# The next head's first scores stand between the third and the fourth turning group of an attention slot

## The reference

```
# q, k, v: 4 batches, 8 heads, 576 positions, 64 wide;  s: 4 x 8 x 576
cum    = cumsum(max(s, 0))
scores = q k^T / 8 + min(-(cum_i - cum_j), 0), causal
attn   = softmax(scores);  o = attn v                  # per head
x = o, heads side by side                              # 2304 tokens x 512
h = x w_in;  solu = h * softmax(h)                     # 2304 x 1024
y = layernorm(solu) * g_ln @ w_out                     # 2304 x 512
out = max(y w1, y w2, y w3) @ w_out2                   # 768 hidden units
```

## Time and profile before

| | |
|---|---|
| median of 3 runs | 727.67 us (727.65 to 728.1) |
| the profiled execution | 727.19 us, span 725.4 us |
| TensorE busy | 705.0 us, 97% of the span |
| VectorE, ScalarE, GpSimd busy | 382.7, 318.4, 258.3 us (53%, 44%, 36%) |
| granted TensorE clock | 0.999 of full speed |
| attention stage | from the start to about 212 us |

### The profile page before, as it was taken

One profiled execution on the slowest core, in us unless ns is written; L12 is line 12 of the kernel. 1 busy time (PEld: TensorE's weight loads), 2 busy tenths in 40 slices (PEclk: granted clock), 3 DMA queues, 4 the chain that ended last, 5 costly groups with the idle time before them and its releaser, 6 DMA issues.

```text
span 725.4 us, 12009 instructions
## 1 busy us (share of the span) xinstructions
PE 705.0 (97%) x4032; PEld 622.3 (86%) x4032; DVE 382.7 (53%) x681; ACT 318.4 (44%) x754; POOL 258.3 (36%) x298
## 2 busy tenths in 40 slices
PE   4899999999999999999999999999999999999998
PEld 3789899888888898989899998888888888888897
DVE  7999999999958656363635545410320132032121
ACT  4889999998964434141414414311211121111121
POOL 8767799999889554342202000000000000000000
PEclk9999999999999999999999999999999999999999
DMA  6577777778575142800000031001000000100000
GB/s 186 159 217 213 205 197 197 196 195 229 144 176 124 43 88 48 215 1 1 1 1 1 3 113 59 0 1 59 0 1 30 29 1 1 58 1 0 30 30 30
DMA packets 57721, 59.52 MB, mean 82 GB/s; under 512 B 23060, under 2 KB 44692, under 8 KB 57652
## 3 DMA queue, kind: packets, MB, share of 16 engines
q1 hardware_dynamic: 57684, 59.02, 30.4%
HBM read 44.15 MB, written 10.10 MB: 75 GB/s over the span
## 4 chain that ended last, share of the span: by engine, by line
PE 84%; DVE 6%; ACT 3%; POOL 3%; issue 3%; DMA 0%; DVEq 0%; POOLq 0%; ACTq 0%; SPq 0%
PE ps L687 10%; PE ps L689 10%; PE ps L688 10%; PE ps L492 6%; PE ps L603 5%; PE ps L605 5%; PE ps L604 5%; PE ps L528 4%; PE ps L530 4%; PE ps L529 4%; PE ps L705 3%; PE ps L707 3%; PE ps L706 3%; PE ps L474 3%; PE ps L500 2%
## 5 line engine op out<-in xcount | busy, mean ns | idle before, releaser
L689 PE MATMUL ps<-x_lo,w_hi 128*128 128x512 f32 (+1 forms) x360 | 132.4, 368 | 0.0
L688 PE MATMUL ps<-x_hi,w_lo 128*128 128x512 f32 (+1 forms) x360 | 132.4, 368 | 0.0
L687 PE MATMUL ps<-x_hi,w_hi 128*128 128x512 f32 (+1 forms) x360 | 132.4, 368 | 0.0
L888 ACT ACTIVATE probs<-ps,nmax 128x576 f32<-128x576 f32 (+4 forms) x160 | 82.8, 537 | 4.5 <-DVE nmax L1090 4.4
L492 PE MATMUL ps<-ident,probs 128*128 128x128 f32 x480 | 75.9, 283 | 5.9 <-DVE pt_lo L1097 2.7
L1097 DVE TENSOR_TENSOR pt_lo<-ps,pt_hi 128x512 fp32r<-128x512 f32 (+2 forms) x128 | 76.2, 636 | 7.9 <-ACT pt_hi L898 5.0
L689 PEld LDWEIGHTS ps<-x_lo,w_hi 128*128 128x128 f32 x360 | 67.9, 189 | 11.3
L688 PEld LDWEIGHTS ps<-x_hi,w_lo 128*128 128x128 f32 x360 | 67.9, 189 | 11.3
L687 PEld LDWEIGHTS ps<-x_hi,w_hi 128*128 128x128 f32 x360 | 67.9, 189 | 11.2
L898 ACT ACTIVATE pt_hi<-ps 128x512 fp32r<-128x512 f32 (+2 forms) x128 | 68.0, 560 | 12.6 <-PE ps L492 9.9
L474 PE MATMUL ps<-k_a,q_a 128*128 128x288 f32 (+2 forms) x192 | 63.4, 338 | 10.4 <-DMA qk_b<-setup 9.8
(11 more groups left out here) (103 smaller groups left out, 1420.6 us busy)
## 6 DMA issues: line engine op xcount, KB each, us to landing
qk_raw<-in_qk_dram SPq DMA_DIRECT2D x32, 576.0 KB, 4.1
xT<-halves SPq DMA_DIRECT2D x32, 144.0 KB, 2.4
xb_dram<-halves SPq DMA_DIRECT2D x32, 144.0 KB, 2.4
xb<-xb_dram SPq DMA_DIRECT2D x24, 192.0 KB, 3.7
rinvB<-rsum_dram SPq DMA_DIRECT2D x24, 192.0 KB, 4.5
stage<-in_moe_w_dram SPq DMA_DIRECT2D x18, 256.0 KB, 4.6
out_dram<-stage SPq DMA_DIRECT2D x18, 256.0 KB, 2.0
v_raw<-in_v_dram SPq DMA_DIRECT2D x32, 128.0 KB, 3.4
```

The lines of the kernel that those rows point to most:

```text
L687: pe.matmul(dst, w_hi[f][:, i, c, :], x2_hi[par][:, c, 0:w], start=(c == 0), stop=False)
L688: pe.matmul(dst, w_lo[f][:, i, c, :], x2_hi[par][:, c, 0:w], start=False, stop=False)
L689: mm = pe.matmul(dst, w_hi[f][:, i, c, :], x2_lo[:, c, CT * g:CT * g + w], start=False, stop=(c == KC - 1))
L888: act.activation(dst, SCORES[c], ACT.Exp, bias=nmax[par][:, c:c + 1], accum_out=sums_all[:, c, bass.ds(t, 1)]).then_inc(exp_done, 1)
```

## The change

S4 now stands between T2 and T3. Its waits for q's high part, k's high part, q's low part, the bias rows and the exp are gone from its head, which keeps only the wait for k's low part (slot 0's own first call and the call for head 1 keep more). Two of those left out, for q's and k's high parts, are implied by the low parts; the other three now stand inside T2, one ahead of each of its second, third and fourth blocks.

```
@@ turn
                 for n, (j, c) in enumerate(blocks):
                     o = chunk_offset(c) + P * j
+                    if g == 2 and n == 1 and live(known, -1):
+                        pe.wait_ge(exp_done, NCH * t + 1)
+                    if g == 2 and n == 2 and live(known, -1):
+                        pe.wait_ge(aux_loaded[1 - par], (t + par) * 8 + 16)
+                    if g == 2 and n == 3 and live(known, -1):
+                        pe.wait_ge(q_lo_ready, t + 2)
                     mm = pe.transpose(ps[:, GBANK[g], P * n:P * (n + 1)], probs[1 - par][:, o:o + P], ident[:, :])
@@ scores_4
-                pe.wait_ge(q_hi_ready, t + 1)
-                pe.wait_ge(k_hi_ready, t + 1)
-                pe.wait_ge(q_lo_ready, t + 1)
                 pe.wait_ge(k_lo_ready, t + 1)
-                pe.wait_ge(aux_loaded[par], (t - par) * 8 + 16)
+                if known is not None and known <= 1:
+                    pe.wait_ge(q_lo_ready, t + 1)
+                    pe.wait_ge(aux_loaded[par], (t - par) * 8 + 16)
                 if known == 0:
                     pe.wait_ge(q_b0_ready, 1)
-                else:
+                elif known == 1:
                     pe.wait_ge(exp_done, NCH * (t - 1) + 1)
@@ slot
                 if live(known, 1):
                     turn(2, t, par, known)
+                if live(known, -1):
+                    scores_4(t + 1, 1 - par, known and known + 1 if known != 0 else 1)
+                if live(known, 1):
                     turn(3, t, par, known)
-                if live(known, -1):
-                    scores_4(t + 1, 1 - par, None)
                 if live(known, 2):
                     values(t, par, 7, PV_B)
```

## The result

The changed kernel takes 740.6 us (740.23 to 740.89), the kernel before 727.66: a ratio of 1.0176, interval 1.0164 to 1.0188, 1.8% slower. The profiled execution has a span of 738.4 us against 725.4, 13.0 more. All of it arises in the attention stage: T0 of slot 3 moves from 29.12 to 29.50, T0 of slot 31 from 199.47 to 212.49. That is 182.99 us for 28 slots, where 170.35 stood.

A forecast was written before the change was run, and what follows sets the result against it. It took T0 to be held by ScalarE's exps, so a later T3 lengthens the slot to 6.35 us: 25 ordinary slots + 8.5, long ones - 0.5, sum + 8.0, giving 735.7 us, range 730.5 to 741.8.

The forecast's parts named there:

- What sets a slot: Attention stage: T0, the next slot's first turning, is held by ScalarE's exps, by 0.09 us; ScalarE has nothing to give.
- The loop, term by term: ScalarE loop from T0 to next T0: 2.84 + 1.08 + 0.54 + 1.86 = 6.32 us, 6.35 with the three waits.
- T0 to T2: TensorE from the first turning's start to the third's: 2.84 us, all of it matmuls back to back.
- T3 to its copy: From the start of turning T3 on TensorE to the start of its pt_hi copy on ScalarE: 0.54 us.
- Copy to T0: From the start of T3's copy on ScalarE, through three exps, to the next slot's T0: 1.86 us.
- the prediction's own sign of being wrong in size: The size would be wrong if T2 with its waits takes more than 0.5 us (among other signs).
- Three waits inside T2: Waits moved between T2's blocks: all for things long done, costing only issue time, 0.03 us for the three.
- waits dear: Rival: the three waits inside T2 cost the full 0.22 us, slot 6.54, total 741.0 us; chance 0.10.
- The six waits at S4's head: The gap ahead of S4's first load: six waits cost 0.22 us together, some 0.04 each.
- Ordinary and long slots: 25 ordinary slots become 6.35 us each, + 8.5; three long ones, 20.10 together, give - 0.5; sum + 8.0.
- GpSimd: It paced the slots in which it also splits w_in, at 6.12 us; these take the new 6.35 too.
- VectorE's longer loop: Rival: from T2 through T3's copy, pt_lo and q_low, 6.15 us, deciding if q_low exceeds 1.4; 741.2; chance 0.07.

The follow-up runs named there:

- e4: The changed kernel with ScalarE doing the three exps ahead of the copy of T3; 740.5 us, ratio 1.0177 against the kernel before.
- e1: The changed kernel with the wait for exp of chunk 4 back at S4's head, not inside T2; 735.37 us, ratio 1.0108 against the kernel before.
- e9: The changed kernel with two waits inside T2 swapped: q_a's low part ahead of the second block, exp of chunk 4 ahead of the fourth; 736.62 us.
- e2: The kernel before with S4 moved ahead of T3 and nothing else, all six waits at S4's head; 737.23 us, ratio 1.0131.
- e6: The kernel before, S4 behind T3, with ScalarE doing the three exps ahead of the copy of T3; 743.27 us, ratio 1.0213.
- e8: The kernel before with ScalarE's exps ahead of the copy of T3 and VectorE's q_low one head further ahead; 729.07 us, ratio 1.0018.
- e7: The changed kernel with exp wait at S4's head, ScalarE's exps ahead of T3's copy, VectorE's q_low one head further ahead; 726.11 us, ratio 0.9988.

## Why the prediction came out as it did

The direction and the loop that sets the slot were right: 735.7 was forecast, in 730.5 to 741.8, with 0.87 on slower; 740.6 came.

- **What sets a slot.** Right for the changed kernel: in its loop slots T0 comes 0.13 to 0.15 behind the last accumulator read and 0.92 to 0.96 behind VB's last matmul. For the kernel before it was read from one slot, and holds in ten of the 24 loop slots. In the other fourteen, all of slots 18 to 27 among them, T0 comes 0.11 or 0.12 behind VB's last matmul, which is TensorE's own pace; in slots 18 to 27 the last read ends 0.16 to 0.22 earlier. ScalarE had some 0.1 us to give there at most, too little to change the sum. e4 shows the hold of the exps as a cause: with the exps freed from the copy of T3, T0 follows VB by 0.11.
- **The loop, term by term.** T0 to T2: forecast 2.84, measured 2.83. S4: 0.66, measured 0.68. T3 to its copy: 0.54, measured 105.79 - 105.26 = 0.53. Copy to T0: 1.86, measured 107.62 - 105.79 = 1.83. T2: forecast 0.42 + 0.03 for the waits, measured 0.62. The sum is 6.49, and only one term was mis-sized. That is the prediction's own sign of being wrong in size, T2 with its waits above 0.5.
- **The term that failed** is "Three waits inside T2. All three are for things long done", and "They cost only issue time", with 0.03. One of them is not for a thing long done. I took from the order on ScalarE that exp of chunk 4 precedes the others and did not set its end beside the new place of the wait. It ends about 3.1 us after T0 (104.22 - 101.13); S4 needs it 3.2 after T0 (e1), but the second block of T2 asks for it at 2.9 already. The gap of 0.19 made the slot 6.50 instead of 6.29, 5.2 us in all (e1). That e1's 735.37 is so near the 735.7 that was forecast is in part luck: without the gap the ordinary slots are 6.29 where 6.35 was forecast, and the long ones and the start make up for it. The time of *waits dear*, 741.0, was nearly hit, but not for its reason: e9 has as many waits and no gap.
- **The six waits at S4's head.** Their 0.22 was read as a price of 0.04 each. e9 shows that a satisfied wait has no fixed price, and the same six cost 0.07 to 0.10 behind T2 (e2), but 0.17 to 0.23 behind T3 in nearly every loop slot of the kernel before, e6 and e8. That T3 had itself just been released from a wait would be a reason, but in three slots of e8 its loads follow T2's without a gap (seven in 0.76 and 0.80), and the gap ahead of S4 is still 0.17 or 0.18. In the one at 56.58 pt_lo of T1 ended at 56.98, only just ahead of T3's first load, so this doesn't settle it; the cause stays open.
- **Ordinary and long slots.** 25 x 6.35 was forecast; they came at (182.99 - 6.52 - 13.97) / 25 = 6.50, + 12.2 instead of + 8.5. The three intervals that were long sum to 6.52 + 13.97 = 20.49 instead of 20.10: one fell to the ordinary length, the two near the end grew. I had - 0.5. Another 0.4 came ahead of slot 3. So of the miss, 3.75 lie in the ordinary slots, 0.9 in the long ones and 0.4 ahead of them.
- **GpSimd** lost its role, as foretold: the slots that were its own are 6.50 like the others.
- **VectorE's longer loop** did not close in the changed kernel: q_low's median fell from 1.21 to 0.76. In e4 and e6 a loop through VectorE closes at 6.42, but another one than was priced: the copy of T3 hangs there on the exps and not on T3. Which loop is next behind ScalarE's in the changed kernel, no run shows.

## What to carry to other kernels

Filling a gap on the busiest engine gains nothing when the work pushed back feeds another engine that has no slack: follow the pushed instruction through the in-order queue of the engine that consumes it, back to where the first engine waits next, and add up that loop. A wait that is moved forward must be held against the time at which its condition comes true, not against the order of issue; moved to a later block, or left at its user, it was free here (e9, e1). And when one loop is opened, the next is close by: here it took two more moves, on ScalarE and VectorE, until the kernel with the earlier S4 was the faster of two, by 3 us, and even that one can't be told from the kernel that all this began with.

## What the runs showed of the hardware that I had not expected

Three satisfied waits between four turnings of 0.1 us each left no gap at all in the weight loads (e9), even with their values computed in the loop. The same six waits left 0.17 to 0.23 us behind T3 (before, e6, e8) and cost 0.07 to 0.10 behind T2 (e2).

And q_low, of fixed size, takes from 0.76 to 1.96 us in these runs, by what GpSimd has under way. Its median in slots 12 to 27 is 1.21 before and in e7, 0.97 in e1, 0.76 in the changed kernel. The time is not simply saved. Fourteen times in a row in the changed kernel, from 93.90 to 178.44, q_low starts 0.10 to 0.13 ahead of GpSimd's low part of k, and that takes about 1.92 us, where its median before is 1.42. The timelines of VectorE and GpSimd:

```profile
106.91 0.76 DVE L1089 SCALAR_TENSOR_TENSOR q_a<-qk_raw,q_a 64x576 fp32r<-64x576 f32 x1
...
107.03 1.90 POOL L756 TENSOR_TENSOR qk_b<-qk_raw,k_a 64x576 fp32r<-64x576 f32 x1
```

Of these two the one that started first kept its length, and the other took 0.5 us longer.
